# Moving the places of on-chip buffers in a three-part kernel: the tokens' parts above the tables, the expert rows and some attention buffers below

## The reference

```python
# 1: attention with a hash mask, 16 heads of 768 x 64
mask = q_bucket[:, :, :, None] == k_bucket[:, :, None, :]
scores = np.where(mask, scale * np.matmul(q, k.transpose(0, 1, 3, 2)), -1e9)
attn = softmax(scores)
x = np.matmul(attn, v)                      # then rearranged to 1536 x 512
# 2: dense mixture: every expert sees every token
P = sinkhorn(exp(x @ w_gate - max))         # 8 rounds over rows and columns
x = sum_e P[:, e:e+1] * (relu(x @ w1[e]) @ w2[e])
# 3: routed mixture: a token goes to one expert
e = argmax(cosine(x, expert_emb) / tau)
out[token] = gate * (relu(x[token] @ m2_w1[e]) @ m2_w2[e])
```

## The kernel before, in words

| buffers | before | after |
|---|---|---|
| ident, ones, tok | 0 to 25,600 | same |
| xt_hi, xt_lo | 25,600 to 74,752 | 98,112 to 147,264 |
| w1_raw, w2_raw | 74,752 to 107,520 | 25,600 to 58,368 |
| gate weights, tables | 107,520 to 112,448 | 93,184 to 98,112 |
| w1_hi, w1_lo | 112,448 to 145,216 | 147,264 to 180,032 |
| w2_hi, w2_lo | 145,216 to 177,984 | 180,032 to 212,800 |
| h_hi, h_lo; g_s, g_row, x_s, w2_raw_even | 177,984 to 210,752 | 58,368 to 91,136 |
| gate_t, x_t | 210,752 to 212,800 | 91,136 to 93,184 |
| attention: q, k, bits, v_s, pt_hi | 112,448 to 176,960 | 147,264 to 211,776 |
| attention: pt_lo, o_t, o_sum, proj_q, proj_k, small columns | 176,960 to 200,832 | 58,368 to 82,240 |
| attention over xt: q_raw, k_raw, v_raw, prob; part 3 over xt: x_row, y_row, diag, hot, tab | inside xt | inside xt |

## Time and profile before

### The profile page before, as it was taken

The page is one execution under the profiler, slowest core; times in us unless marked ns, Lnnn a source line. Parts: engine busy times, 40 slices in busy tenths (PEclk is TensorE's granted clock), DMA queues, the critical chain, the costliest instruction groups (busy, mean ns, idle before and its releaser), DMA issues.

```text
span 1584.9 us, 21759 instructions
## 1 busy us (share of the span) xinstructions
PE 1565.8 (99%) x7562; PEld 1303.9 (82%) x7563; DVE 684.9 (43%) x1235; ACT 510.9 (32%) x932; POOL 333.5 (21%) x563
## 2 busy tenths in 40 slices
PE   9999999999999999999999999999999999999997
PEld 8999997888888888888888888888888887788886
DVE  7888886433221211212322121121232255887665
ACT  6887885112111100111211110011121123576554
POOL 4565556100300300020030030003004000232222
PEclk9999999999999999999999999999999999899999
DMA  6555561100200110110020011011002121674310
GB/s 160 135 119 144 134 187 54 54 0 31 77 1 1 55 51 0 53 53 0 16 90 0 0 53 53 0 53 53 0 3 103 41 80 74 221 272 158 130 43 25
DMA packets 45095, 109.97 MB, mean 69 GB/s; under 512 B 5750, under 2 KB 7798, under 8 KB 45056
## 3 DMA queue, kind: packets, MB, share of 16 engines
q1 hardware_dynamic: 41408, 100.91, 20.6%
q0 software_dynamic: 3424, 8.14, 1.6%
q10 hardware_dynamic: 224, 0.39, 0.1%
HBM read 81.57 MB, written 8.13 MB: 57 GB/s over the span
## 4 chain that ended last, share of the span: by engine, by line
PE 97%; DVE 1%; ACT 1%; issue 0%; POOL 0%; DVEq 0%; POOLq 0%; ACTq 0%
PE psum L463 27%; PE psum L465 26%; PE psum L464 26%; PE psum L768 4%; PE psum L755 2%; PE psum L782 2%; PE psum L781 2%; PE psum L756 2%; PE psum L735 1%; PE psum L1095 1%; PE psum L795 1%; PE psum L902 1%; PE psum L1086 0%; PE psum L703 0%; DVE pt_lo L1406 0%
## 5 line engine op out<-in xcount | busy, mean ns | idle before, releaser
L1277 ACT ACTIVATE h_hi<-psum 128x512 fp32r<-128x512 f32 x192 | 114.9, 598 | 889.1 <-PE psum L465 889.1
L463 PE MATMUL psum<-xt_lo,w_hi 128*128 128x512 f32 x768 | 304.1, 396 | 0.0
L464 PE MATMUL psum<-xt_hi,w_hi 128*128 128x512 f32 x768 | 302.7, 394 | 0.0
L465 PE MATMUL psum<-xt_hi,w_lo 128*128 128x512 f32 x768 | 302.7, 394 | 0.0
L463 PE MATMUL psum<-w_lo,h_hi 128*128 128x512 f32 x768 | 302.3, 394 | 0.0
L465 PE MATMUL psum<-w_hi,h_lo 128*128 128x512 f32 x768 | 299.2, 390 | 0.0
L464 PE MATMUL psum<-w_hi,h_hi 128*128 128x512 f32 x768 | 299.2, 390 | 0.0
L1702 DVE SCALAR_TENSOR_TENSOR h_lo<-psum,h_hi 128x512 fp32r<-128x512 f32 x192 | 132.9, 692 | 366.2 <-ACT h_hi L1277 366.2
L494 POOL CAST w_hi<-w_raw 128x512 fp32r<-128x512 f32 x68 | 41.5, 611 | 811.2 <-PE psum L465 810.8
L1765 DVE SCALAR_TENSOR_TENSOR tok<-psum,route,tok 128x512 f32<-128x512 f32 x83 | 56.8, 745 | 354.9 <-PE psum L465 354.9
L465 PEld LDWEIGHTS psum<-xt_hi,w_lo 128*128 128x128 f32 x768 | 143.7, 187 | 35.4
(11 more groups left out here) (270 smaller groups left out, 2024.7 us busy)
## 6 DMA issues: line engine op xcount, KB each, us to landing
w_raw<-in_moe_w_dram SPq DMA_DIRECT2D x25, 2048.0 KB, 8.4
w_raw_odd<-in_moe_w_dram SPq DMA_DIRECT2D x4, 2048.0 KB, 11.6
k_hh<-k_hi SPq DMA_DIRECT2D x32, 192.0 KB, 3.0
w_raw_even<-in_moe_w_dram SPq DMA_DIRECT2D x3, 2048.0 KB, 8.5
x_rows<-tok SPq DMA_DIRECT2D x14, 256.0 KB, 2.4
k_raw<-in_k_dram SPq DMA_DIRECT2D x8, 384.0 KB, 3.1
v_raw<-in_v_dram SPq DMA_DIRECT2D x16, 192.0 KB, 3.5
k_b<-k_lo SPq DMA_DIRECT2D x15, 192.0 KB, 3.3
```

The source lines that it names most:

```text
L463: pe.matmul(acc, a[0], b[1], start=start, stop=False)
L464: pe.matmul(acc, a[0], b[0], start=False, stop=False)
L465: return pe.matmul(acc, a[1], b[0], start=False, stop=stop)
L1277: act.activation(h_s[0][:, f, :], psum[:, f % 4, :], ACT.Relu).then_inc(m1.h_hi, 1)
```

## The change

The tokens' parts xt_hi and xt_lo, with everything that lies over them, move from just behind tok to behind the tables, ahead of w1 and w2. The raw weights move down into their place. The expert rows (h_s, and with them g_s, g_row, x_s, w2_raw_even), gate_t and x_t move from the top to behind the raw weights. The attention buffers from pt_lo on are placed from there, too. Two assertions change with this. No instruction, wait, shape or order changes.

```diff
--- before.py
+++ after.py
@@ -63,11 +63,15 @@
     ones = place("ones", [P, P], F32)
     turned = top[0]
     tok = place("tok", [P, TT, DM], F32)
-    dead = top[0]
-    xt = [place("xt_hi", [P, KD, N], F32R), place("xt_lo", [P, KD, N], F32R)]
     x_nat = tok[:].rearrange("p a b -> p (a b)")[:, 0:TT * DM].rearrange("p (n t d) -> p n t d", n=NH // 2, t=IT)
     w1_raw = place("w1_raw", [P, KD, FF], F32)
     w2_raw = place("w2_raw", [P, KF, DM], F32)
+    h_at = top[0]
+    h_s = [place("h_hi", [P, KF, 512], F32R), place("h_lo", [P, KF, 512], F32R)]
+    gate_t_at = [top[0]]
+    gate_t = place("gate_t", [2 * E, 512], F32)
+    x_t = place("x_t", [P, KD, P], F32, gate_t_at)
+    emb_sq = gate_t[0:E, :]
     gate_at = [top[0]]
     gate_w16 = place("gate_w16", [P, KD, 2 * E], F32R)
     gate_raw = place("gate_raw", [P, KD, E], F32)
@@ -105,17 +109,13 @@
     block_i = place("block_i", [P, TT], I32, cell_at)
     id_i = place("id_i", [P, TT], I32, cell_at)
     emb_raw = place("emb_raw", [E, DM], F32, tables)
+    dead = top[0]
+    xt = [place("xt_hi", [P, KD, N], F32R), place("xt_lo", [P, KD, N], F32R)]
     shared = top[0]
     assert shared % 64 == 0 and dead % 64 == 0
 
     w1_s = [place("w1_hi", [P, KD, FF], F32R), place("w1_lo", [P, KD, FF], F32R)]
     w2_s = [place("w2_hi", [P, KF, DM], F32R), place("w2_lo", [P, KF, DM], F32R)]
-    h_at = top[0]
-    h_s = [place("h_hi", [P, KF, 512], F32R), place("h_lo", [P, KF, 512], F32R)]
-    gate_t_at = [top[0]]
-    gate_t = place("gate_t", [2 * E, 512], F32)
-    x_t = place("x_t", [P, KD, P], F32, gate_t_at)
-    emb_sq = gate_t[0:E, :]
 
     w2_p = [[[x[:, f // 2, f % 2 * 512:f % 2 * 512 + 512] for f in range(KF)] for x in xt],
             [[w[:, f, :] for f in range(KF)] for w in w2_s]]
@@ -160,6 +160,8 @@
     v_s = [place(f"v_s{u}", [P, IT, 2 * D], F32R, at) for u in range(2)]
     prob = [place(f"prob{u}", [P, IT, P], F32, beside[3 + u]) for u in range(2)]
     pt_hi = [place(f"pt_hi{u}", [P, IT, HALF], F32R, at) for u in range(2)]
+    assert at[0] <= shared + 4 * KD * FF * 4
+    at = [h_at]
     pt_lo = [place(f"pt_lo{u}", [P, IT, HALF], F32R, at) for u in range(2)]
     o_t = place("o_t", [P, HALF], F32, at)
     o_sum = [place(f"o_sum{u}", [P, IT // 2, D], F32, at) for u in range(2)]
@@ -176,7 +178,7 @@
     row_sum = place("row_sum", [P, 2 * IT], F32, at)
     row_den = place("row_den", [P, 2 * IT], F32, at)
     row_inv = place("row_inv", [P, 2 * IT], F32, at)
-    assert at[0] <= nc.sbuf_usable_end
+    assert at[0] <= h_at + 2 * KF * 512 * 4
 
     psum = nc.alloc_psum_tensor("psum", [P, 8, 512], F32)
```

## The result

| | before | after |
|---|---|---|
| median | 1586.88 us (4 runs, 1586.04 to 1587.43) | 1576.39 us (4 runs, 1575.51 to 1577.01) |
| the profiled execution, its span | 1586.95, 1584.9 us | 1576.39, 1574.3 us |

The ratio is 0.9932, with a 95% interval of 0.992 to 0.9944: 10.5 us less, where 15.1 were forecast. The measured time lies inside the range, but 4.2 us above the 1572.2 that were forecast. Among all executions in this document one stands apart: one of the ten of experiment 5 took 4009.41 us, for a reason that the record doesn't show; the nine others took 1585.18 to 1587.12, and their median alone is 1586.80.

The account below looks back on a forecast made before the run. PE bounds the kernel (97% of the span), through its start-to-start matmul distance. Terms -15.4 - 0.9 - 0.1 + 1.3 = -15.1 us, from the median 1587.31 to 1572.2 us; range 1570.6 to 1579.0.

Parts of the forecast that it names:

- The forecast is wrong if down-projections move at all: Sign in the timeline: 96 down matmuls should stay at 21.8 us while 96 up matmuls fall from 22.4 to 21.8.
- the kind of stage: Alternative explanation of 233.3 against 226.9 ns, excluded because part 3's same instruction took 233 or 227 ns by w2's place.
- The place of the streamed operand goes with the 6.67 ns: PE matmuls of 512 columns: streams at 74,752 or below start 6.67 ns further apart than those at 112,448 or above.
- Item 1: Up-projections, xt moved up: 2304 matmuls each 6.67 ns shorter, -15.4 us; held stages might keep 3.2 us.
- Item 2: Part 3 with w2 over xt, 144 matmuls, -0.9 us; the gate, 24 matmuls, -0.1 us.
- Item 3: Attention, pt_lo moved down and streamed: 192 matmuls each pay 6.67 ns, +1.3 us, lower bound 0.
- Item 4: h, g and x_s moved down as weights in parts 2 and 3: taken as 0, bounds 0 and 6.67 ns per matmul.
- item 5: prob and x_row moved up as weights of transposes: taken as 0, at most 1.2 us of gain.
- (b): Stream and weights on different sides (low, high) cost the step, so down-projections lengthen: +5.8, 1593.1 us, chance 0.12.
- (d): Half the gain: both operands' places count with parts of a step, or POOL or DVE slow; 1578 to 1586, chance 0.05.
- (a): No effect: something accompanying the place causes the 6.67 ns, up-projections keep 233 ns; 1587.3 us, chance 0.08.
- (c): Low region ends inside xt_hi, so its first blocks keep 233 ns; up to 1578.5 us, chance 0.09.

Follow-up runs that it names:

- experiment 5: Kernel before with 192 bytes of tables (reach, emb_t) placed ahead of xt, so xt begins at 25,792; 1586.93 us, ratio 0.9998.
- experiment 4: Kernel before with one 64-byte table (reach) placed ahead of xt, so xt begins at 25,664; 1571.39 us, ratio 0.9905.
- experiment 1: Changed kernel with the tables (4,928 bytes) ahead of h instead of behind x_t, moving h, g and x_s up; 1571.92 us, ratio 0.9907.
- experiment 2: Kernel before with the tables (4,928 bytes) ahead of xt instead of behind the raw weights; 1571.28 us, ratio 0.9903.
- experiment 3: Changed kernel with the tables behind w2, so xt, w1, w2 and h begin on multiples of 128; 1571.45 us, ratio 0.9903.
- experiment 11: Experiment 4 with attention's k_hh and k_b placed 192 bytes further on than q_t and q_b; 1571.41 us, ratio 0.9907.
- experiment 9: Experiment 2 with one 64-byte table (reach) between w2 and h instead, moving h, g and x_s 64 bytes on; 1588.45 us, ratio 1.0011.
- experiment 7: Experiment 3 with 64 bytes of tables on either side of w1_lo, which also moves w2 by 128 against h; 1596.73 us, ratio 1.0064.
- experiment 6: Experiment 3 with 64 bytes of tables ahead of xt and 64 between xt and w1, moving w2 by 128 against h; 1600.26 us, ratio 1.0084.

## Why the prediction was right, and where it was not

The time fell into the range, but partly by luck, and by the prediction's own sign the forecast was wrong: "The forecast is wrong if down-projections move at all", and they moved by 0.20 us each.

**What bounds the kernel: right.** PE's distance from start to start was what moved, and no other engine became late. The reading of 233.3 and 226.9 ns out of the earlier trace rows and the exclusion of "the kind of stage" by the earlier trace rows hold: experiment 4 moves xt alone by 64 bytes, and both the up-projection's 22.40 us (to 21.76) and the median distance behind xt_hi,g_hi in part 3 (from 233 to 227 ns) fall.

**"The place of the streamed operand goes with the 6.67 ns": the property was the wrong one.** The step needs both operands. In the kernel before, the weights of all the big products (w1, h, x_s, g_s, v_s) happened to have one phase, so that the stream's place alone seemed to decide. The text saw the second difference between the classes (multiples of 128 or 64 past one) and left region and phase open, but it took both as properties of the stream. Experiments 1 to 3 show that neither is: what counts is the difference, and experiments 4 and 5 give the modulus, 256.

**Item 1, up-projections: right, by 15.4 us.** The reason given was not the one at work, though: the new xt happened to agree with w1 modulo 256.

**Item 2, part 3 over xt and gate, -0.9 and -0.1: not seen.** Part 3 as a whole stayed at 205.6 to 205.7 us. The tiles over xt lost their difference of -64 but got +64 against g_s, and so did the other products of part 3, against x_s and g_s. A gain of 0.9 us could hardly be seen there in any case: experiments 1 and 2, with all differences of part 3 at 0, have 206.0 and 204.8 us for it. The gate's 23 distances take 5.31 to 5.32 us in every kernel here. Its four blocks of weights (kd) lie 64 bytes apart, so that each kernel has all four differences in its gate, wherever xt lies.

**Item 3, pt_lo, +1.3: measured 0.** The difference was -64 there, and 384 columns don't pay it (experiment 11). The step was taken from 512 columns without a row at 384 that had it.

**Item 4, weights moved down, taken as 0: the step that failed.** It measured 24 x 0.20 = 4.8 us, inside the bounds of 0 and 15.4 but not at the end that was chosen. The two rows that it leaned on say little: the weight load takes 188 ns in both stages of the changed kernel, too, though a down-projection is 0.2 us longer there, so its duration doesn't tell; and the transposes, with 128 columns, have a median distance of 109 ns in both kernels, though with this change their difference went from 0 to -64 (which bears out the 0 of item 5). The gate's 231.3 ns, named under rival (b), were no hint either, by what item 2 says of them. No row of the kernel before had the weights of a big product at another phase, so its trace could not have given this price.

**The sum:** -15.4 + 4.8 = -10.6, as measured; the forecast's sum differs by item 4 (+4.8), item 3 (-1.3) and item 2 (+1.0).

**The rivals.** (b) was right that the pair decides and wrong in its mechanism (regions) and price: the down-projection's difference was +64, which costs a third of -64. With -64 there, experiment 9 (differences 0 and -64) comes out 0.11% slower than the kernel before (interval 0.01 to 0.21%, some 2 us), where (b) said 5.8 us. The first case of (d), "both the stream's and the weights' place count with parts of a step", is nearest to what happened; the measured time is 1.6 us outside its interval of 1578 to 1586. (a) and (c) fell: up-projections moved, and evenly. The range held the time because (c), a case that was not true, had stretched it upward: its other reason, 3.2 us for stages that are held, ends at 1575.4, below the measured 1576.39. That is luck.

The Trainium skill, "TensorE: Matmul & The Clock Gate", "Part 2: What happens when you issue a matmul", says that the next weights' load takes nothing from the running matmul, since the two have separate read ports. That can't be all there is to it here: moving the weights alone (experiment 1) changes the distance from 228.9 to 226.7 ns, though no run shows whether it is the load that does it. What in the chip makes the difference modulo 256 matter was not found out.

## What to carry to other kernels

Where 512-column fp32r matmuls with new weights each time stand back to back, compare their start-to-start distance between stages; if it differs by 2 to 7 ns, work out each operand's address modulo 256 and place streamed operand and weights alike, which may take no more than moving one small table. Let every big operand's size be a multiple of 256, assert the agreement in the code, and check all pairs at once, as a buffer moved for one product is the partner in another. Other types, and matmuls that keep their weights, were not tried. A cost that goes with a place in one trace leaves open which property of the place it is, and whose; a shift of 64 bytes costs one run and separates region from phase.

## What the runs showed that was not expected

- The distance of 512-column matmuls depends on stream minus weights modulo 256: 226.7 ns at 0; 228.9 to 229.1 at 64; 232.3 to 233.3 at 128; 233.3 at 192 and at 32. 0, 64, 128 and 192 were each seen in both stages. 0, 128 and 192 were each seen at two phases of the operands themselves, 64 and 32 at one only.
- It is not symmetric: +64 costs one step of 16 clocks for three matmuls, -64 one for each, on average.
- One odd operand among three costs two steps, not one (experiment 7).
- At 384 columns the same combination costs nothing measurable (experiment 11).
- With the same places of both operands a down-projection took 22.30 us in experiment 6 and 22.40 in experiment 7.
- Four layouts with both differences at 0 (experiments 1 to 4), in different regions, agree within 0.7 us (1571.28 to 1571.92), 5 us better than the change and 15 better than the kernel before.
